# Two changes to the order of an attention, Fourier and MLP kernel: where a feature transform stands, and how and when batch 1's mean is formed

## What is computed

```
attention: 8 heads of 64, decaying linear attention, in chunks -> x [2, 768, 512]
X = fft(fft(x, axis=1), axis=2);  u = x + real(X)
mu = mean(u, axis=-1);  var = mean((u - mu) ** 2, axis=-1)
un = (u - mu) / sqrt(var + 1e-6)
x3 = u + maximum(un @ w_ch1, 0) @ w_ch2          # 512 -> 2048 -> 512
gate = sigmoid(depthwise causal convolution of x3, 5 taps)
out = (gate * (x3 @ w_val)) @ w_out
```

## Time and profile before

| what | value |
|---|---|
| median of 3 runs | 435.31 us (435.11 to 436.54) |
| the profiled execution: time, span of its instructions | 435.0 us, 433.3 us |
| PE busy (matmuls) | 425.3 us, 98% |
| DVE, ACT, POOL busy | 59%, 35%, 34% |
| granted TensorE clock | 1.00 of full speed |
| chain that ended last: PE, DVE | 91%, 5% |

### The profile page before, as it was taken

One profiled execution on the slowest core, in us unless ns is written; L12 is line 12 of the kernel. 1 busy time (PEld: TensorE's weight loads), 2 busy tenths in 40 slices (PEclk: granted clock), 3 DMA queues, 4 the chain that ended last, 5 costly groups with the idle time before them and its releaser, 6 DMA issues.

```text
span 433.3 us, 7138 instructions
## 1 busy us (share of the span) xinstructions
PE 425.3 (98%) x2912; PEld 408.0 (94%) x2912; DVE 254.8 (59%) x438; ACT 152.0 (35%) x288; POOL 146.2 (34%) x101
## 2 busy tenths in 40 slices
PE   7899999999999999999999999999999999999997
PEld 6787888999999999999999999999999999989986
DVE  5648998772349635435334249938567559889120
ACT  1353442653212411115333253552242261615222
POOL 3543442565342225223754522342242291000000
PEclk9999999999999999999999999999999999999999
DMA  7887500241211303020311202303202200001112
GB/s 247 324 318 245 196 2 5 97 123 71 97 34 65 98 0 98 0 98 2 98 48 51 97 17 82 98 0 98 97 2 97 93 6 2 1 2 73 73 50 97
DMA packets 12560, 35.73 MB, mean 82 GB/s; under 512 B 1648, under 2 KB 1904, under 8 KB 12528
## 3 DMA queue, kind: packets, MB, share of 16 engines
q1 hardware_dynamic: 12528, 35.28, 24.1%
HBM read 32.13 MB, written 3.15 MB: 81 GB/s over the span
## 4 chain that ended last, share of the span: by engine, by line
PE 91%; DVE 5%; DMA 1%; issue 1%; ACT 0%; POOL 0%; SPq 0%; DVEq 0%; POOLq 0%
PE ps L541 10%; PE ps L543 10%; PE ps L564 10%; PE ps L563 10%; PE ps L562 10%; PE ps L542 10%; PE ps L634 3%; PE ps L635 3%; PE ps L633 3%; PE ps L657 3%; PE ps L656 3%; PE ps L655 3%; PE ps L412 2%; PE ps L470 1%; PE ps L450 1%; PE ps L495 1%
## 5 line engine op out<-in xcount | busy, mean ns | idle before, releaser
L745 ACT ACTIVATE hh<-ps 128x384 fp32r<-128x384 f32 x64 | 31.4, 493 | 170.7 <-PE ps L543 170.7
L1020 DVE SCALAR_TENSOR_TENSOR hl<-ps,hh 128x384 fp32r<-128x384 f32 x64 | 35.3, 557 | 90.5 <-ACT hh L745 90.5
L541 PE MATMUL ps<-cen_h,w1h_a 128*128 128x384 f32 x128 | 43.8, 343 | 0.0
L541 PE MATMUL ps<-cen_h,w1h_b 128*128 128x384 f32 x128 | 43.7, 341 | 0.0
L543 PE MATMUL ps<-cen_h,w1l_b 128*128 128x384 f32 x128 | 43.2, 338 | 0.0
L564 PE MATMUL ps<-hh,w2l_b 128*128 128x384 f32 x128 | 43.2, 337 | 0.0
L562 PE MATMUL ps<-hh,w2h_b 128*128 128x384 f32 x128 | 43.2, 337 | 0.0
L563 PE MATMUL ps<-hl,w2h_b 128*128 128x384 f32 x128 | 43.1, 337 | 0.0
L543 PE MATMUL ps<-cen_h,w1l_a 128*128 128x384 f32 x128 | 43.1, 337 | 0.0
L542 PE MATMUL ps<-cen_l,w1h_a 128*128 128x384 f32 x128 | 43.1, 337 | 0.0
L542 PE MATMUL ps<-cen_l,w1h_b 128*128 128x384 f32 x128 | 43.0, 336 | 0.0
(11 more groups left out here) (168 smaller groups left out, 998.5 us busy)
## 6 DMA issues: line engine op xcount, KB each, us to landing
raw_a<-in_mlp SPq DMA_DIRECT2D x16, 512.0 KB, 4.7
raw_b<-in_mlp SPq DMA_DIRECT2D x16, 512.0 KB, 4.4
chunks<-in_qkv SPq DMA_DIRECT2D x12, 512.0 KB, 6.6
chunks<-in_qkv SPq DMA_DIRECT2D x22, 256.0 KB, 6.1
out<-out_sb SPq DMA_DIRECT2D x11, 256.0 KB, 2.0
raw_a<-in_val SPq DMA_DIRECT2D x2, 512.0 KB, 4.5
raw_b<-in_out SPq DMA_DIRECT2D x2, 512.0 KB, 4.6
seq_c<-const_seq SPq DMA_DIRECT2D x1, 768.0 KB, 7.9
```

The costliest lines, as they stand in the source:

```text
L541: mm(bank, wh_, xh, start=r == 0, stop=False)
L745: nc.scalar.activation(hh[:, slot, j], ps[j][:, 0:TB], ACT.Relu).then_inc(s_hh, 1)
L1020: stt(hl[:, slot, j], ps[j][:, 0:TB], 0.0, hh[:, slot, j].bitcast(F32), ALU.max, ALU.subtract).then_inc(s_hl, 1)
```

## The change

1. In phase A, chunk 6 (`n == NC`): PE issues `from_chunk(6)` ahead of `hid_transform(5)` and no longer behind it. Other chunks keep the old order.
2. `mean(1)`: `usum` is first split in a rounded part and a rest. ACT rounds it (`sum_hi`) and DVE subtracts (`sum_lo`), both in step 10. PE then uses two fp32r matmuls for each half of the tokens (four in all) in place of one fp32 matmul for each.
3. `mean(1)` stands behind step 11 in place of step 10. `centre` moves to step 12, `cen_hi` to 12 and 13, `squares` to 14 and 15, and DVE's `cen_lo` to 13 and 14. `squares_hi`, the variance and all of POOL's order stay where they were.

```diff
@@ mean
-                pe.wait_ge(s_sum, (R - 1) * (b + 1))
                 pe.wait_ge(s_u, added_u(b, R - 1))
+                if b == 0:
+                    pe.wait_ge(s_sum, R - 1)
+                else:
+                    pe.wait_ge(s_mh, 1)
+                    pe.wait_ge(s_ml, 1)
                 for hf in range(2):
-                    mm(ps[(COS, SIN)[hf]][:, 0:TB], ones[:, :], usum[:, hf * TB:(hf + 1) * TB],
-                       start=True, stop=True).then_inc(s_mean, 1)
+                    bank, cols = ps[(COS, SIN)[hf]][:, 0:TB], slice(hf * TB, (hf + 1) * TB)
+                    if b == 0:
+                        mm(bank, ones[:, :], usum[:, cols], start=True, stop=True).then_inc(s_mean, 1)
+                    else:
+                        mm(bank, ones_r[:, :], square_part[1][:, 0, cols], start=True, stop=False)
+                        mm(bank, ones_r[:, :], square_part[1][:, 1, cols], start=False, stop=True).then_inc(s_mean, 1)
@@ PE, attention loop
-                if 1 <= n <= NC:
+                if 1 <= n < NC:
                     hid_transform(n - 1)
                 if n:
                     from_chunk(n)
+                if n == NC:
+                    hid_transform(n - 1)
@@ PE, mlp_step
-                if st.m == 10:
+                if st.m == 11:
                     mean(1)
@@ ACT
+            def sum_hi():
+                act.wait_ge(s_sum, 2 * (R - 1))
+                act.wait_ge(s_f, 2 * R * B)
+                copy(square_part[1][:, 0], usum).then_inc(s_mh, 1)
...
-                if st.m in (11, 12):
-                    cen_hi(1, st.m - 11)
-                if st.m in (13, 14):
-                    squares(1, st.m - 13)
+                if st.m == 10:
+                    sum_hi()
+                if st.m in (12, 13):
+                    cen_hi(1, st.m - 12)
+                if st.m in (14, 15):
+                    squares(1, st.m - 14)
@@ DVE
+            def sum_lo():
+                dve.wait_ge(s_mh, 1)
+                tt(square_part[1][:, 1], usum, square_part[1][:, 0].bitcast(F32), ALU.subtract).then_inc(s_ml, 1)
...
-                if st.m == 11:
+                if st.m == 10:
+                    sum_lo()
+                if st.m == 12:
                     centre(1, 0)
                     centre(1, 1)
-                if st.m in (12, 13):
-                    cen_lo(1, st.m - 12)
+                if st.m in (13, 14):
+                    cen_lo(1, st.m - 13)
```

## The result

The changed kernel took 439.25 us (median of 6 runs, 438.64 to 440.16), the kernel before 435.79 us beside it (435.02 to 436.7). The ratio is 1.0085, 95% interval 1.0068 to 1.0102: slower by 3.7 us (3.0 to 4.4). The direction was forecast, the size was not: +2.15 us were forecast, and the range ended at 438.4.

A forecast was written before the change was run, and what follows sets the result against it. PE, busy for all 330 us from 90 to 420 us, bounds phases B and C; 0 - 0.58 + 2.73 = +2.15 us on the 435.31 us median gives 437.4 us. The range of 8 in 10 was 436.2 to 438.4.

The forecast's parts named there:

- Edit 1 is worth nothing: Phase A, chunk 6: from_chunk put ahead of the feature transform; forecast 0, with bounds of -0.78 and +0.24 us.
- The mean, -0.58 us: Phase B, mean(1): four fp32r matmuls at 0.71 us replace the fp32 mean at 1.29 us, a gain of 0.58 us.
- The stall of 2.73 us: Near 224 us PE's mlp_hidden(16) waits for DVE's second cen_lo, queued behind step 14's add_mlp and held by POOL: +2.73 us.
- the exclusion: DVE's late cen_lo is blocked until POOL's square_sum instruction ends; rival without it: stall 1.79 us, sum +1.21, chance 0.13.
- The clock falls in the stall: Rival: PE's 2.7 us gap before mlp_hidden(16) brings back half clock, 1.2 GHz; sum +4.0, 439.3 us, chance 0.07.

## Why the prediction was wrong

- **Edit 1 is worth nothing: right**, and for the reason given. Alone it measures 0.9996, and `two_odd` takes 0.68 us when POOL is away.
- **The mean, -0.58 us: right.** 0.70 us for four matmuls by the trace; two kernels that keep it and avoid the stall are 0.65 and 0.7 us faster than before, the second with an interval that reaches no change.
- **The stall of 2.73 us: right.** 2.69 by the trace, with its parts: 0.47 us from `add_mlp` to `cen_lo`, POOL 0.8 us ahead, the end 0.81 us behind POOL's. The kernel that moved the square sum shows that the exclusion is what lifts the stall from 1.79 us. The trace of before had more such cases than the two that the prediction used, and they agree: `cen_lo` at 80.24 us and two instructions of 768 columns at 298.11 and 314.89 ended 0.82 to 0.83 us behind POOL's.
- **"The clock falls in the stall", chance 0.07: this was the failing step.** I kept the forecast, the sum without it, at 0.61. It happened in every run of the changed kernel, and the forecast is short by its cost. The argument was that PE had never been idle for more than 1.5 us in the trace, at full granted clock. But the earlier trace rows begins at 90 us, behind that gap, which lies at 12 us, and a gap of 1.5 us without a fall says only that 1.5 us did no harm there. For 2.7 us no row spoke on either side, and then 0.07 was an opinion. The price in the rival was off too, 1.9 us for 1.53, since I took the length of the stretch from the kernel's start (3.78 us) and doubled the spacing; it lasted about 3.5 us (227.54 to 231.02), with the spacing at 0.32 us, 1.84 times that of full clock. The row from the start was a weak base: the granted clock there reads 1.00, and the slow stretch is not of one length: the 16 matmuls of `scores` behind the row took 2.08 us in one execution and 1.16 in the other.
- **The range.** It had its upper end 1 us above the forecast and left out the one case that stood above, 439.3 us. With the clock at an even chance, as the missing rows would have allowed, it would have reached it. That the measured 439.25 us falls on this case is in part luck: its price for the clock was about 0.36 us too high, and the kernel before measured 435.79 us beside it, 0.48 above the 435.31 that the sum started from.

The Trainium skill's warning, "TensorE: Matmul & The Clock Gate", section "Why this matters for your kernels", that an idle gap between matmuls returns the engine to half rate, was weighed and put aside for want of a row. The trace now agrees with it, and shows the fall behind 2.0 and 2.4 us of idle time, gaps that this section would still let pass.

## What to carry to other kernels

Before moving a step, look for what its last instruction stands behind in its engine's queue: an instruction that waits for the very block ahead of its reader turns a slack of ten microseconds into a stall, and one place earlier costs nothing. A gap in PE's stream beyond the longest that the trace shows unharmed should be priced with the clock's fall as a likely case and not as a tail. Filling idle time of an engine helps only if the engine that ends the stage moves too; here POOL's hold on DVE took the time back at once.

## What the runs showed of the hardware

- Behind 2.42 us of idle time on PE the granted clock fell to 1.2 GHz in 6 of 6 runs, behind 1.99 us in 6 of 7, behind 1.51 us in 0 of 12 at the same place. Elsewhere in the program, with several gaps near each other and the longest 1.5 us, it fell in 2 of 12, and with the longest 2.1 us in 10 of 12. The gaps are those of one trace each. So no sharp length holds for all places.
- The fall comes after the gap: 0.8 us into the resumed matmuls with 2.42 us of idle time, 1.35 us with 1.99. It cost 1.5 to 1.6 us in both.
- At half clock a stream of 128x384 fp32r matmuls runs at 0.32 us each, at full clock at 0.17.
- A DVE instruction of 768 columns with both inputs in SBUF that is issued inside a POOL instruction ends 0.81 to 0.83 us behind it, where its own time is 0.95. The traces of before, of the changed kernel and of the two with matmuls in the gap show nineteen such cases.
